# Spreading the dispatch scatters over the attention's quarters, with a third rounding buffer, another order of the first maxima and of the weight, query, key and value loads

## What is computed

```python
scores = where(mask, q @ k.T / 8, -1e9)
attn = exp(scores - scores.max(-1)); attn /= attn.sum(-1) + 1e-9
x = (attn @ v).transpose(0, 2, 1, 3).reshape(2304, 512)

e = argmax(x @ w_gate, 1); gate = softmax(x @ w_gate)[e]
pos = rank of the token within its expert, kept if pos < capacity
x = gate * (relu(x @ w1[e]) @ w2[e])          # 0 if not kept

e2 = argmax(x @ w_gate2, 1); gate2 = softmax(x @ w_gate2)[e2]
out = x + (x @ w_skip > 0) * gate2 * (relu(x @ w1b[e2]) @ w2b[e2])
```

## Time and profile before

| what | before |
|---|---|
| median of the runs | 683.83 us (683.19 to 685.59) |
| the profiled execution, its own time | 684.36 us |
| its span, first to last instruction | 682.8 us |
| mean granted TensorE clock | 0.995 |
| PE busy / weight loads / DVE / ACT / POOL | 97% / 85% / 54% / 43% / 29% of the span |
| DMA queue of SP and ACT: packets, MB | 84608, 81.03 |
| DMA queue of POOL: packets, MB | 8912, 22.36 |

### The profile page before, as it was taken

How to read it: one execution, slowest core, us unless ns; L and a number is a source line. 1 busy time by engine, 2 the same in 40 slices (tenths; PEclk the granted TensorE clock), 3 DMA queues, 4 the chain that set the end, 5 groups by cost and what they waited for, 6 DMA issues and landing times.

```text
span 682.8 us, 17206 instructions
## 1 busy us (share of the span) xinstructions
PE 662.0 (97%) x5640; PEld 580.6 (85%) x5641; DVE 371.4 (54%) x1029; ACT 290.7 (43%) x713; POOL 195.7 (29%) x329
## 2 busy tenths in 40 slices
PE   7999998998998999999999999999999999999997
PEld 6788887887887888989889988888899899899996
DVE  4777886886886663357733357433812453411144
ACT  4678775776775212244412244213321352411133
POOL 6523344235234122322223212123112122112112
PEclk9999999999999999999999999999999999999999
DMA  9866676555615147611521048893265778701101
GB/s 190 205 165 192 168 179 199 129 127 163 153 24 166 39 150 245 247 34 38 207 94 46 31 138 315 300 325 113 107 235 179 264 287 301 275 31 46 46 18 33
DMA packets 95616, 105.91 MB, mean 155 GB/s; under 512 B 63757, under 2 KB 63757, under 8 KB 95568
## 3 DMA queue, kind: packets, MB, share of 16 engines
q1 hardware_dynamic: 84608, 81.03, 38.2%
q0 software_dynamic: 8912, 22.36, 9.8%
q10 hardware_dynamic: 2048, 1.87, 0.8%
HBM read 83.44 MB, written 28.63 MB: 164 GB/s over the span
## 4 chain that ended last, share of the span: by engine, by line
PE 93%; DVE 2%; issue 2%; ACT 1%; another core or an unknown queue 0%; DVEq 0%; POOL 0%; ACTq 0%; POOLq 0%
PE ps L1551 33%; PE ps L1559 26%; PE ps L1446 7%; PE ps L1397 6%; PE ps L1421 5%; PE ps L1453 4%; PE ps L1373 3%; PE ps L1523 2%; PE ps L1387 2%; PE ps L1529 1%; PE ps L1414 1%; PE ps L1537 1%; DVE negmax L799 1%; PE ps L1364 1%; ACT probs L1217 0%
## 5 line engine op out<-in xcount | busy, mean ns | idle before, releaser
L1551 PE MATMUL ps<-xT,w 128*128 128x128 f32 x1344 | 159.6, 276 | 1.7 <-issue 1.5
L1551 PEld LDWEIGHTS ps<-xT,w 128*128 128x128 f32 x1344 | 155.0, 192 | 5.9 <-issue 3.9
L1559 PE MATMUL ps<-w_hi,hT_hi 128*128 128x512 f32 x256 | 104.7, 409 | 0.7 <-DVE hT_lo L1068 0.7
L1559 PE MATMUL ps<-w_lo,hT_hi 128*128 128x512 f32 x256 | 100.3, 392 | 0.0
L1559 PE MATMUL ps<-w_hi,hT_lo 128*128 128x512 f32 x256 | 99.7, 389 | 0.0
L1278 ACT ACTIVATE hT_hi<-ps 128x512 fp32r<-128x512 f32 x64 | 38.0, 593 | 115.9 <-PE ps L1551 114.4
L1551 PE MATMUL ps<-xT,w_last 128*128 128x128 f32 x704 | 86.3, 277 | 0.0
L1551 PEld LDWEIGHTS ps<-xT,w_last 128*128 128x128 f32 x704 | 82.3, 192 | 3.0 <-issue 2.2
L1068 DVE SCALAR_TENSOR_TENSOR hT_lo<-ps,hT_hi 128x512 fp32r<-128x512 f32 x64 | 44.2, 691 | 63.1 <-ACT hT_hi L1278 59.7
L1273 ACT ACTIVATE w_hi<-w2all 128x1024 fp32r (+1 forms) x48 | 47.0, 1046 | 62.6 <-PE ps L1559 56.7
L533 POOL DMA_INDIRECT out<-xs,idxo x32 | 37.4, 1169 | 110.1 <-DVE xs L1101 102.5
(11 more groups left out here) (200 smaller groups left out, 1026.0 us busy)
## 6 DMA issues: line engine op xcount, KB each, us to landing
w2all<-in_moe_w SPq DMA_DIRECT2D x10, 2048.0 KB, 15.1
w<-in_moe_w SPq DMA_DIRECT2D x7, 2048.0 KB, 9.5
rows<-queue POOLq DMA_DIRECT2D x36, 257.0 KB, 3.0
w2all<-in_moe_w SPq DMA_DIRECT2D x16, 512.0 KB, 4.6
w<-in_moe_w SPq DMA_DIRECT2D x12, 512.0 KB, 3.6
w_last<-in_moe_w SPq DMA_DIRECT2D x3, 2048.0 KB
qn<-in_q SPq DMA_DIRECT2D x32, 144.0 KB, 5.2
out<-pad SPq DMA_DIRECT2D x4, 1152.0 KB
```

The costliest lines, as they stand in the source:

```text
L1551: last = mm(hTp[j // 4][:, j % 4, :], w1s[slot][:, c, j * P:(j + 1) * P], xT[:, c, :], start=(c == 0), stop=(c == DC - 1))
L1559: last = mm(yp, h_[:, j, :].bitcast(f32r), w_[:, j, :].bitcast(f32r), start=(j + n == 0), stop=(j == FC - 1 and n == 2))
```

## The change

Five things, all in the attention's part; PE's program is the same.

- POOL: `scatter_batch` becomes `scatter_tile`. For the first two batches the first scatter stands behind quarter 3 of pairs 7 and 11, the other four behind the four quarters of pairs 8 and 12, and the wait for all five with the token numbers two quarters later. Before the copy of the last block of pairs 8 and 12 POOL waits for the first three scatters to have landed. The third batch's first scatter stands behind quarter 3 of pair 15, and its other four directly behind it, with no wait. The last batch is as before.
- ACT and POOL: three `whole` buffers, so that ACT waits for the quarter three before.
- DVE at the begin: two remainders, the maxima of step 0, two remainders, the maxima of step 1.
- SP: queries three pairs ahead in a pair's third step, keys in its fourth, values one pair ahead in its second, a weight quarter in its first (and in its second for pairs 2, 5, 9, 13), each behind a wait for `pv_ready` of that step.
- SP: the second weights of expert 0 come first, then its first weights; the zeros for the output go in the fourth step of pairs 3, 6, 10 and 13.

```diff
-    QUICK = 2
+    QUICK, WHOLES = 2, 3
...
-        whole = [sba(f"whole{i}", [P, S // 2]) for i in range(2)]
+        whole = [sba(f"whole{i}", [P, S // 2]) for i in range(WHOLES)]
...
             load_qk(1)
+            sp.wait_ge(qk_transposed, 4)
+            load_qk(2)
             sp.dma_start(wg2[:, :, 0:E], ...
...
+            load_v(1)
+            pieces = [(load_quarter_w2, 0, u) for u in range(NPAIR)] + [(load_quarter_w1, 0, u) for u in range(NPAIR)]
+            pieces += [(load, 1, u) for load in (load_quarter_w1, load_quarter_w2) for u in range(NPAIR)]
+            pieces += [(load_quarter_w1, 2, u) for u in range(NPAIR)]
+            PIECES_AT = sorted([(p, 0) for p in range(PAIRS)] + [(p, 1) for p in (2, 5, 9, 13)])
+            CLEARS_AT = [(3, 3), (6, 3), (10, 3), (13, 3)]
+            for pair in range(PAIRS - 1):
+                for n in range(STEPS):
+                    at = (pair, n)
+                    if pair + n:
+                        sp.wait_ge(pv_ready, STEPS * pair + n)
+                    if at in PIECES_AT:
+                        load, e, u = pieces[PIECES_AT.index(at)]
+                        load(e, u)
+                    if n == 1 and pair:
+                        load_v(pair + 1)
+                    if n > 1 and pair + 3 < PAIRS:
+                        if n == 2:
+                            sp.wait_ge(qk_transposed, 4 * (pair + 2))
+                        load_qk(pair + 3, ((q, qn, q_loaded) if n == 2 else (k, kn, k_loaded),))
+                    if at in CLEARS_AT:
...
+            sp.wait_ge(pv_ready, STEPS * (PAIRS - 1))
+            load, e, u = pieces[-1]
+            load(e, u)
...
-            def scatter_batch(b):
+            def scatter_tile(b, i):
...
-                for i in range(NI):
-                    scatter(queue1, xs[b % 2][:, i, :], idxq[:, i:i + 1], TAIL - 1, scattered)
-                if b < B - 1:
-                    pool.wait_ge(scattered, (b + 1) * (NI * 16))
+                scatter(queue1, xs[b % 2][:, i, :], idxq[:, i:i + 1], TAIL - 1, scattered)
...
                         if part == 2:
+                            if pair > NPAIR and pair % NPAIR == 0:
+                                pool.wait_ge(scattered, (pair // NPAIR - 2) * (NI * 16) + 3 * 16)
                             copy_qlast(pair)
...
+                        b = pair // NPAIR - 1
+                        if 0 <= b and pair % NPAIR == NPAIR - 1 and part == 3:
+                            scatter_tile(b, 0)
+                        if 1 <= b and pair % NPAIR == 0:
+                            scatter_tile(b - 1, part + 1)
+                        if 1 <= b and pair % NPAIR == 1 and part == 1 and b + 1 < B:
+                            pool.wait_ge(scattered, b * (NI * 16))
+                            write_tokens(b + 1)
+            for i in range(1, NI):
+                scatter_tile(B - 2, i)
...
-            for part in range(4):
-                split_qk(0, part)
-            step_max(0)
-            step_max(1)
+            for half in range(2):
+                for part in range(2 * half, 2 * half + 2):
+                    split_qk(0, part)
+                step_max(half)
...
-                if pair >= QUICK and i - 2 >= 4 * QUICK:
-                    act.wait_ge(qk_split, i - 1)
+                if pair >= QUICK and i - WHOLES >= 4 * QUICK:
+                    act.wait_ge(qk_split, i - WHOLES + 1)
```

More of the change, by code:

```diff
@@ L354, in _ @@
                          allow_slow_non_contiguous=True).then_inc(consts_loaded, 16)
-            for pair in range(PAIRS):
-                b, u = pair // NPAIR, pair % NPAIR
-                if pair + 2 < PAIRS:
-                    sp.wait_ge(qk_transposed, 4 * (pair + 1))
-                    load_qk(pair + 2)
-                if pair + 1 < PAIRS:
-                    if pair:
-                        sp.wait_ge(pv_ready, STEPS * pair)
-                    load_v(pair + 1)
-                if b < WSLOT - 1:
-                    load_quarter_w1(b, u)
-                if b < WSLOT - 2:
-                    load_quarter_w2(b, u)
-                if u == NPAIR - 1:
-                    if b == 0:
-                        sp.wait_ge(pad_made, 1)
-                    sp.dma_start(out.rearrange("(o p j) d -> o p j d", o=B, j=XJ)[b, :, :, :],
-                                 pad[0:XP, 0:D].unsqueeze(1).to_broadcast([XP, XJ, D])).then_inc(out_cleared, 16)
+            load_v(1)
@@ new lines, in _ @@
+            pieces = [(load_quarter_w2, 0, u) for u in range(NPAIR)] + [(load_quarter_w1, 0, u) for u in range(NPAIR)]
[3 more added lines that the diff above has]
+            CLEARS_AT = [(3, 3), (6, 3), (10, 3), (13, 3)]
+            assert len(PIECES_AT) == len(pieces)
@@ new lines, in _ @@
+            for pair in range(PAIRS - 1):
[13 more added lines that the diff above has]
+                    if at in CLEARS_AT:
+                        part = CLEARS_AT.index(at)
+                        if part == 0:
+                            sp.wait_ge(pad_made, 1)
+                        sp.dma_start(out.rearrange("(o p j) d -> o p j d", o=B, j=XJ)[part, :, :, :],
+                                     pad[0:XP, 0:D].unsqueeze(1).to_broadcast([XP, XJ, D])).then_inc(out_cleared, 16)
@@ L487, in split_qk @@
                 pool.wait_ge(qk_rounded, i + 1 - 4 * QUICK)
-                g.tensor_tensor(lo[par][:, cols].bitcast(f32r), whole[i % 2][:, :], hi[par][:, cols], ALU.subtract).then_inc(qk_split, 1)
+                g.tensor_tensor(lo[par][:, cols].bitcast(f32r), whole[i % WHOLES][:, :], hi[par][:, cols], ALU.subtract).then_inc(qk_split, 1)
             copy_qlast(0)
@@ L534, in scatter @@
                                         bounds_check=last_row, oob_is_err=False).then_inc(done, 16)
[L536 to L545 removed]
+            def scatter_tile(b, i):
+                if i == 0:
+                    if b == 0:
+                        pool.wait_ge(first_padded, 16 * (2 * FIRSTS - 1))
+                        pool.wait_ge(placed, 16)
+                    pool.wait_ge(indices_ready, b + 1)
+                scatter(queue1, xs[b % 2][:, i, :], idxq[:, i:i + 1], TAIL - 1, scattered)
             def write_tokens(b):
@@ L561, in _ @@
                         if part == 2:
+                            if pair > NPAIR and pair % NPAIR == 0:
+                                pool.wait_ge(scattered, (pair // NPAIR - 2) * (NI * 16) + 3 * 16)
                             copy_qlast(pair)
-                if pair % NPAIR == NPAIR - 1 and pair > NPAIR:
-                    b = pair // NPAIR - 1
-                    scatter_batch(b)
-                    if b + 2 < B:
-                        write_tokens(b + 2)
+                        b = pair // NPAIR - 1
[8 more added lines that the diff above has]
+                scatter_tile(B - 2, i)
             for phase in range(2):
@@ L616, in _ @@
                     pool.wait_ge(p.first_loaded[1], 16)
-                    scatter_batch(B - 1)
+                    for i in range(NI):
+                        scatter_tile(B - 1, i)
                 pool.wait_ge(p.rows_ready, 1)
@@ L1191, in copy_qk @@
                 hi = (qT_hi, kT_hi)[which][par][:, cols].bitcast(f32r)
-                if pair >= QUICK and i - 2 >= 4 * QUICK:
-                    act.wait_ge(qk_split, i - 1)
-                to = hi if pair < QUICK else whole[i % 2][:, :]
+                if pair >= QUICK and i - WHOLES >= 4 * QUICK:
+                    act.wait_ge(qk_split, i - WHOLES + 1)
+                to = hi if pair < QUICK else whole[i % WHOLES][:, :]
                 if which == 0:
@@ L1200, in copy_qk @@
                     act.wait_ge(qk_copied, i + 1)
-                    sc.activation(hi, whole[i % 2][:, :], ACT.Copy).then_inc(qk_rounded, 1)
+                    sc.activation(hi, whole[i % WHOLES][:, :], ACT.Copy).then_inc(qk_rounded, 1)
             def router_exp(R, begin, done, value):
```

4 lines of the change are left out of this document (removed).

## The result

The change is slower. Its median is 688.68 us (687.88 to 688.78, 5 runs) against 683.83 us (682.39 to 685.59, 5 runs) in the same group of runs: the ratio is 1.0067, interval 1.0052 to 1.0082. The forecast was 679.8 us and its range ended at 685.2. The profiled execution of the change took 687.88 us, its span is 686.3 us, 3.5 more than before.

A forecast was written before the change was run, and what follows sets the result against it. The prediction took PE to bound the kernel (93% of the chain that ended last). Its terms, -6.35 + 1.1 + 1.2 = -4.05 us, took the median from 683.83 to 679.8 us, range 676.0 to 685.2.

The forecast's parts named there:

- Scatters spread: Attention, first two batches: without five scatters back to back, the bursts with late signals go; -6.35 us.
- Single scatters: Attention: six lone scatters beside query or key loads each still hold PE up 0.18 us; +1.1 us.
- Third batch: After pair 15's last quarter: five scatters stay in a row, PE loses 1.97 us and clock as before; 0.
- cured too: Rival: the third batch's burst also loses its wait, as SP's queue is lighter there; 676.1 us, chance 0.13.
- New wait before the last-block copy: POOL, pairs 8 and 12: waiting for three landed scatters costs 0, with over 3 us of cover.
- Third buffer: ACT and POOL: a third whole buffer helps only where POOL is over a step late; 0.
- First maxima: Attention's begin: remainders behind step 0's maxima delay step 1's exponentials, and the shift stays; +1.2 us.
- clock fall: Rival: PE idling 2.0 us at the begin lowers its clock, up to +1.7 us; 681.5 us, chance 0.12.
- Loads: SP's queue: later queries and keys land in time, zeros only delay the scatters' landing, which has cover; 0.
- The scatters are not the cause: Rival: something else in those steps makes signals late, so the bursts' 6.35 us remain; 685.0 us, chance 0.12.
- Single scatters hold signals as well: Rival: each of ten scatters costs up to 0.89 us, slower from 0.52 us each; 687.6 us, chance 0.13.

The follow-up runs named there:

- e9: The kernel before with only the scatters spread (old loads, zeros, two whole buffers, old first maxima); 674.72 us, ratio 0.9851.
- e19: e17 run once more in a later group of runs; 679.18 us, ratio 0.9919.
- e14: e9 run once more, unchanged, in a later group; 676.46 us, ratio 0.988.
- e17: e9 with one scatter less ahead of the last-block copy, whose wait asks for two tiles in place of three; 675.7 us, ratio 0.9856.
- e12: The kernel before run once more, unchanged, for its trace; 685.13 us, ratio 0.9996.
- e13: The change run once more, unchanged; 689.2 us, ratio 1.0064.
- e10: e2 with the old first maxima and two whole buffers in place of three; 680.38 us, ratio 0.9929.
- e4: The kernel before with only the new order of first remainders and maxima; 685.28 us, ratio 1.0018.
- e15: The change with the second and third batch's zeros one step later, behind the third scatter; 680.67 us, ratio 0.9939.
- e16: e9 with the second and third batch's zeros where the change has them, ahead of the third scatter; 679.74 us, ratio 0.9917.
- e8: e2 with the old first maxima and the second batch's zeros put back to the fourth step of pair 6; 681.78 us, ratio 0.9959.
- e2: The change with the zeros of two batches a whole pair earlier, in pairs 5 and 9; 682.86 us, ratio 0.9983.

## Why the prediction was wrong

- *Scatters spread, -6.35 us.* Right in the main where it was read: against e9's pairs 6 and 7, and 10 and 11, in place of pairs 2 and 3, the loss was 5.97. Alone, with one scatter less before the copy, it gave -4.7 us where signals are late (e19), against -6.35 + 1.1 = -5.25 forecast. Without late signals it gave 9 to 10 us (e9, e14, e17), by the mechanism of e12 as well, which the text set aside: "ACT and POOL need not be behind for that". True of that trace, not of every execution.
- *Single scatters, +1.1 us.* Under-sized for the change. Between marks pairs 6 and 10 took 13.84 and 13.91 us against 12.8, so 1.0 to 1.1 a batch, 2.1 in all, of which PE's four waits for ACT's copies are 1.7; with the old loads it was 0.2 to 0.5 a batch (e19), and without late signals 0 (e13). The mark 0.52 us each, from which that rival decides, was not reached.
- *Third batch, 0.* Right: five in a row still hold signals up when any scatter does (e19). Rival "cured too" is out.
- ***New wait before the last-block copy, "0, with over 3 us of cover". This step failed***, and with it the sentence on the zeros under loads, that sharing the queues "only delays their landing, which has the cover above". Two errors lie in it. The cover is 2.5 us. And the landing was never priced: the term counted from the issue of the scatter, one step before, as if it landed in that step. It took 7.5 and 9.0 us. The text named both halves, 1152 KB of zeros on the scatters' queues and a wait for the scatters' landing, and set each to 0 by the other. That the next split and scatter would queue behind the wait on POOL was described rightly. The path from there was not: it was to reach PE through a full `whole` buffer and ACT, three quarters later, but ACT never waited for POOL. PE waited for the very next remainder, and so the cover is shorter. PE's two waits took 5.1 us and the clock behind them about 3.0; with the 2.1 us above that is 10.2, where the marks show 9.8. No rival priced it.
- *Third buffer, 0.* Right: the cover is 2.5 us with two (e10) and with three (e13).
- *First maxima, +1.2 us.* Right: 1.03 us in the trace, 1.2 us (0.4 to 2.1) in e4. That rival's clock fall did not come in the change's trace (1.00 over 8 to 20 us, behind a wait of 1.84); it is seen in 14 of the 20 traces, with the old maxima too (0.86 in e9's), so the order does not decide it.
- *Loads, 0.* Wrong for the zeros: ahead of the third scatter they cost 4.5 us of POOL's waits (e13 beside e15) and made most of the failure above. No load reached PE late in the change's trace. The queries, keys and weights one kind a step cost 2 to 4.5 us of POOL's waits where no signal was late; what they cost in the first trace stays open.
- *Rivals.* "The scatters are not the cause" fell with e9. The Trainium skill's rule behind it ("SBUF — State Buffer", section "Who interferes with whom") is about data ports, and no run here speaks against it: what the runs show is a matter of queue order and of signals. "Single scatters hold signals as well" came within 1.1 us of the measured time (687.6), for another reason. That it was near is luck: it had the side right by the wrong mechanism.

## What to carry to other kernels

A wait for a DMA to land is priced by what is queued ahead of it, not by when it was issued; before adding one, list what every queue issues in the two steps before, and move the large transfers that nobody waits for behind it. Where such a transfer gets a wait of its own, look at what stands behind it in the same queue: it is held too, as the queries were in e16. When one part of a change makes a wait and another makes what it waits for slower, two zeros are not a sum of zero. And one profile can hide the second mechanism behind the first: the kernel before loses its time behind the scatters in two quite different ways, in different executions.

## What the runs showed of the hardware

- The late signals come and go with the occasion. The first traces, the first group and the fifth have them in every kernel with scatters in the attention; the twelve kernels of the second to fourth groups have none in these pairs that an engine waits for. In the spread batches they are short: four waits of PE, 1.7 us in the change's trace, 1.3 in e2's. The second and the fifth group ran on one chip. What sets them off stays open.
- A 257 KB scatter issued 1.0 to 1.4 us after 1152 KB of zeros had landed by 7.5 to 10.1 us later, in five cases (the change's two traces, e8); issued 0.8 us ahead of them, by 6.8 us later (e15); issued 3.3 to 3.8 us ahead of them, with the old loads, by 4.0 to 5.4 us later (e9, e14).
- Behind waits of PE of 1.84, 1.97 (before) and 3.25 to 4.95 us the granted clock fell to 0.50, 1.2 of 2.4 GHz (e8, the stretch in which PE starts again, below). Behind 1.72 and 1.82 us (e15, e10) it did not, and neither behind 2.83 us in e12, where it did behind 3.50. So the length of the wait alone does not tell.

```profile
119.00:120.00 1.00, 0.74 (x4) 0.74 (x6) 0.00 (x0) 0.00 (x0) 0.84 (x2) 0.50 0.59 226
```
